# Routing logits on VectorE from replicated gate columns, k double-buffered, q and v single, and the last first-layer weights queued ahead of block 1

## What is computed

```python
# local attention: chunks of 32 queries, 16 keys to the left, 8 to the right, 8 memory keys
scores = scale * np.matmul(q_c, k_full.transpose(0, 1, 3, 2))
a = np.exp(scores - np.max(scores, axis=-1, keepdims=True))
a = a / (np.sum(a, axis=-1, keepdims=True) + 1e-09)
out[:, :, c_start:c_end] = np.matmul(a, v_full)
# dense feed-forward layer, 512 -> 2048 -> 512
h = x @ w_in
x = (h * (1.0 / (1.0 + np.exp(-h)))) @ w_out
# routed layer, 8 experts, one per token
logits = x @ w_gate + modality_bias[modality_id]
e_idx = np.argmax(logits, axis=1)
gate_w = softmax(logits)[e_idx]
out[mask] = gate_w * (np.maximum(x[mask] @ w1[e], 0.0) @ w2[e])
```

## Time and profile before

| | |
|---|---|
| median of 3 runs | 1012.25 us (1011.86 to 1015.44) |
| the profiled execution's own time | 1014.22 us |
| its span, first to last instruction | 1012.6 us |
| TensorE clock granted, mean share | 0.994 |
| TensorE, VectorE, ScalarE, GpSimd busy | 96%, 31%, 35%, 30% |

### The profile page before, as it was taken

How to read it: one execution, slowest core, us unless ns; L and a number is a source line. 1 busy time by engine, 2 the same in 40 slices (tenths; PEclk the granted TensorE clock), 3 DMA queues, 4 the chain that set the end, 5 groups by cost and what they waited for, 6 DMA issues and landing times.

```text
span 1012.6 us, 18134 instructions
## 1 busy us (share of the span) xinstructions
PE 976.3 (96%) x6148; PEld 842.9 (83%) x6149; DVE 309.1 (31%) x749; ACT 354.6 (35%) x728; POOL 302.9 (30%) x318
## 2 busy tenths in 40 slices
PE   4799999999999999999999999999999999999997
PEld 3688889889888888988888898988788888888875
DVE  4422323232422332332422221347332422222221
ACT  5655343343343343333344322343322322222221
POOL 4677222322232322232232234241122222222222
PEclk9999999999999999999999999998999999999999
DMA  7831021212322141242121002232511111111111
GB/s 265 306 105 55 25 78 40 71 47 72 65 47 79 57 57 40 63 49 78 56 56 55 1 33 63 83 94 33 199 54 37 44 38 42 42 42 42 42 42 44
DMA packets 31257, 69.35 MB, mean 68 GB/s; under 512 B 5343, under 2 KB 9439, under 8 KB 31168
## 3 DMA queue, kind: packets, MB, share of 16 engines
q1 hardware_dynamic: 22064, 48.29, 17.0%
q0 software_dynamic: 5904, 13.57, 4.5%
q10 hardware_dynamic: 3200, 6.34, 2.0%
HBM read 55.43 MB, written 13.02 MB: 68 GB/s over the span
## 4 chain that ended last, share of the span: by engine, by line
PE 91%; DMA 3%; DVE 2%; issue 1%; ACT 1%; POOL 1%; ACTq 0%; SPq 0%; POOLq 0%; DVEq 0%
PE bank L1261 26%; PE bank L1247 25%; PE bank L1458 14%; PE bank L1327 13%; PE bank L1232 2%; PE bank L1208 2%; PE bank L1469 2%; DMA q_in<-q_t 2%; PE bank L1292 2%; PE bank L1218 1%; PE bank L1316 1%; PE bank L1275 1%; DMA token_lists<-token,slot 1%; DVE row_sum L888 0%; ACT q_bd L637 0%
## 5 line engine op out<-in xcount | busy, mean ns | idle before, releaser
L578 POOL TENSOR_TENSOR g_lo<-g_raw,g_hi 128x384 fp32r<-128x384 f32 x128 | 131.3, 1026 | 412.0 <-ACT g_hi L771 400.5
L734 ACT ACTIVATE sig<-bank 128x384 f32<-128x384 f32 x128 | 62.8, 491 | 352.2 <-PE bank L1247 352.1
L904 DVE SCALAR_TENSOR_TENSOR g_raw<-sig,bank 128x384 f32<-128x384 f32 x128 | 70.9, 554 | 368.8 <-ACT sig L734 359.0
L1247 PE MATMUL bank<-x_hi,w_hi 128*128 128x384 f32 x512 | 177.7, 347 | 0.0
L1247 PE MATMUL bank<-x_hi,w_lo 128*128 128x384 f32 x512 | 173.2, 338 | 0.0
L1247 PE MATMUL bank<-x_lo,w_hi 128*128 128x384 f32 x512 | 172.1, 336 | 1.1 <-issue 1.1
L1261 PE MATMUL bank<-w_hi,g_hi 128*128 128x512 f32 x384 | 157.0, 409 | 3.1 <-POOL g_lo L578 3.1
L1261 PE MATMUL bank<-w_hi,g_lo 128*128 128x512 f32 x384 | 151.3, 394 | 0.0
L1261 PE MATMUL bank<-w_lo,g_hi 128*128 128x512 f32 x384 | 151.0, 393 | 0.0
L1247 PEld LDWEIGHTS bank<-x_hi,w_hi 128*128 128x128 f32 x512 | 96.5, 189 | 5.2
L1247 PEld LDWEIGHTS bank<-x_lo,w_hi 128*128 128x128 f32 x512 | 96.6, 189 | 3.2
(11 more groups left out here) (165 smaller groups left out, 1253.3 us busy)
## 6 DMA issues: line engine op xcount, KB each, us to landing
k_in<-k_ctx SPq DMA_DIRECT2D x32, 384.0 KB, 4.2
v_in<-v_ctx SPq DMA_DIRECT2D x32, 384.0 KB, 3.2
w_raw<-w SPq DMA_DIRECT2D x8, 1024.0 KB, 5.7
token_rows<-y_sb ACTq DMA_DIRECT2D x8, 774.0 KB, 3.9
q_in<-q_t SPq DMA_DIRECT2D x32, 192.0 KB, 3.1
w_raw<-w_in SPq DMA_DIRECT2D x4, 1024.0 KB, 6.9
w_raw<-w_out SPq DMA_DIRECT2D x4, 1024.0 KB, 8.6
list_id<-token_lists POOLq DMA_DIRECT2D x28, 0.5 KB, 2.3
```

The lines of the kernel that those rows point to most:

```text
L578: eng.tensor_tensor(g_lo[:, f % 2, :], g_raw[:, f % 2, :], g_hi[:, f % 2, :].bitcast(F32), ALU.subtract).then_inc(g_split, 1)
L734: eng.activation(sig[:, f % 2, :], h_bank[f % 2][:, 0:BLOCK], ACT.Tanh, scale=0.5)\
L904: eng.scalar_tensor_tensor(out=g, in0=s, scalar=1.0, in1=h_bank[f % 2][:, 0:BLOCK], op0=ALU.add, op1=ALU.mult).then_inc(g_done, 1)
L1247: mm = eng.matmul(h_bank[f % 2][:, 0:BLOCK], a, b, start=(k == 0 and n == 0), stop=(k == KC - 1 and n == 2))
```

## The change

- The routing logits of blocks 0 to 6 are computed by VectorE: `score(it, n)` multiplies a tile of y with one gate column that is replicated over all partitions (`wg_rows`, 128 x 8 x 512) and sums over the 512 elements, in one instruction and an accumulator read. There are 24 of them (3 tiles, 8 experts) in each of `it` = 2 to 8, three in each slot 3 to 10, each waiting for the one before, and they stand ahead of `silu` of their slot. `transpose_y`, `move_yt` and `logits` remain for the last block alone.
- `x_raw` is gone. `rest_of_x` moves from GpSimd to VectorE, which reads `o_bank` itself, behind `silu` of slots 3, 6, 9, 12; `values` waits for it (`x_split`) instead of for `x_hi_done`.
- `sig` is gone: tanh is written into `g_raw`, so it waits for the `g_lo` of two slots before (`g_split`) where `silu` did.
- q and v have one buffer (in block 0 parts of `wg_rows` serve as the second), k keeps two. Loads go in the order k, q of the next pair, then v of this one (`load_ahead`).
- Weight chunks 4 to 7 are queued ahead of the waiting loads of block 1, and behind those comes the load of `wg_rows`, 16 KB into each of 128 partitions (2 MB written).
- Some small tiles move to other memory, so `move_pt(0)` waits for `zero_stored` and `move_y` of `it` = 2 for `lists_cleared`.

The core of the diff:

```diff
-        q_in = early("q_in", [P, 2, BLOCK])
+        q_in = early("q_in", [P, BLOCK])
         k_in = early("k_in", [P, 2, CHUNKS * KEYS])
-        v_in = early("v_in", [P, 2, CHUNKS * HEAD_DIM])
+        v_in = early("v_in", [P, CHUNKS * HEAD_DIM])
+        wg_rows = early("wg_rows", [P, EXPERTS, D])
...
+        def pairs_before(blk, p):
...
+            return blk * PAIRS + p - (1 if blk * PAIRS + p <= PAIRS else 0)
...
             def load_q(blk, p):
-                need(eng, q_ready, 2 * (blk * PAIRS + p) - 2)
+                need(eng, q_ready, pairs_before(blk, p) * 2)
...
             def load_v(blk, p):
-                need(eng, pv_done, blk * PAIRS + p - 1)
+                need(eng, pv_done, pairs_before(blk, p))
...
-            load_v(1, 0)
-            load_pairs((1, 1),)
             for c in range(PAIRS, 2 * CHUNKS_W):
                 load_first(c)
+            load_ahead(1, 0)
+            eng.wait_ge(pv_done, PAIRS)
+            eng.dma_start(wg_rows[:, :, :], w_gate_t.partition_broadcast(P)).then_inc(rows_known, 16)
...
                 eng.wait_ge(pv_done, u + 1)
-                need(eng, x_split, u)
-                eng.activation(x_raw[:, :], o_bank[:, 0:BLOCK], ACT.Copy)
                 need(eng, l1_done, (it - 1) * FC)
                 eng.activation(x_hi[:, par, p, :], o_bank[:, 0:BLOCK], ACT.Copy).then_inc(x_hi_done, 1)
...
                         eng.wait_ge(l1_done, i + 1)
-                        need(eng, g_done, i - 1)
...
-                        eng.activation(sig[:, f % 2, :], h_bank[f % 2][:, 0:BLOCK], ACT.Tanh, scale=0.5)\
+                        need(eng, g_split, i - 1)
+                        eng.activation(g_raw[:, f % 2, :], h_bank[f % 2][:, 0:BLOCK], ACT.Tanh, scale=0.5)\
...
+            def rest_of_x(it, p, par):
+
+                eng.wait_ge(x_hi_done, it * PAIRS + p + 1)
+                eng.tensor_tensor(x_lo[:, par, p, :], o_bank[:, 0:BLOCK], x_hi[:, par, p, :].bitcast(F32), ALU.subtract)\
+                   .then_inc(x_split, 1)
...
+            def score(it, n):
+
+                t, e = divmod(n, EXPERTS)
+                if e == 0:
+                    eng.wait_ge(y_moved, (it - 2) * TT + (t + 1))
...
+                ins = eng.tensor_tensor_reduce(products[:, :], y_sb[:, t, 0:D], wg_rows[:, e, :], 1.0, 0.0, ALU.mult, ALU.add,
+                                               scored[:, t, e:e + 1])
+                ins.then_inc(score_step, 1)
...
+                    if route and ffn and 3 <= f < 3 + EXPERTS:
+                        for n in range((f - 3) * TT, (f - 2) * TT):
+                            score(it, n)
                     if route and f == 11:
                         route_choice(it)
...
                     if ffn:
                         silu(i, f)
+                    if attn and 1 <= p <= PAIRS and third == 0:
+                        rest_of_x(it, p - 1, par)
...
-                need(eng, x_hi_done, u)
+                need(eng, x_split, u)
...
-                    for t in tiles_at(it, f, 5) if route else ():
+                    for t in last_tiles(it, f, 5):
                         logits(it, t)
...
-                    for t in tiles_at(it, f, 3) if route else ():
+                    for t in last_tiles(it, f, 3):
                         transpose_y(it, t)
```

More of the change, by code:

```diff
@@ L247, in steps, with last_tiles @@
             step(BLOCKS + 1, 1, False, False, True, False)
[L249 to L253, removed]
+        def last_tiles(it, f, at):
+            return range(TT) if isinstance(it, int) and it == BLOCKS + 1 and f == at else ()
         def yt_bank(it, t):
-            return (pt_bank, *h_bank)[t] if isinstance(it, int) and it == BLOCKS + 1 else pt_bank
+            return (pt_bank, *h_bank)[t]
         def first_pieces(f):
@@ L274, in prob_of, with q_of, v_of @@
         def prob_of(it, p):
-            return y_t[:, 0, 0:TT, :].rearrange("p k s -> p (k s)") if doubled(it, p) else prob[:, :]
+            return wg_rows[:, 1, 0:BLOCK] if doubled(it, p) else prob[:, :]
+        def q_of(it, p):
+            return wg_rows[:, 0, 0:BLOCK] if doubled(it, p) else q_in[:, :]
+        def v_of(it, p):
+            return wg_rows[:, 2:4, :].rearrange("p e n -> p (e n)")[:, 0:CHUNKS * HEAD_DIM] if doubled(it, p) else v_in[:, :]
+        def pairs_before(blk, p):
+            if not isinstance(blk, int):
+                return blk * PAIRS + p
+            return blk * PAIRS + p - (1 if blk * PAIRS + p <= PAIRS else 0)
         def piece(to, i):
@@ L385, in _, with load_ahead @@
             load_first(3)
[L387 to L391, removed]
+            def load_ahead(blk, p):
+                if p < PAIRS - 1:
+                    load_k(blk, p + 1)
+                    load_q(blk, p + 1)
+                else:
+                    load_k(blk + 1, 0)
+                    load_q(blk + 1, 0)
+                load_v(blk, p)
             eng.dma_start(ids_sb[:, :, :], ids).then_inc(consts_loaded, 16)
@@ L470, in _ @@
             eng.memset(y_sb[:, :, D + 1:ROW], 0.0).then_inc(consts_made, 1)
-            eng.memset(zero_row, 0.0).then_inc(pool_step, 1)
             eng.iota(pad_ids, pattern=[[0, LIST // P]], base=PAD_TOKEN, channel_multiplier=0).then_inc(pool_step, 1)
-            eng.wait_ge(pool_step, 6)
+            eng.wait_ge(pool_step, 5)
             eng.dma_start(rows[TOKENS:TOKENS + 1, :], zero_row).then_inc(zero_stored, 16)
             eng.dma_start(lists.rearrange("(p n) a -> p (n a)", p=P), pad_ids).then_inc(lists_cleared, 16)
[L479 to L484, removed]
             def list_tokens(it, t):
@@ L748, in step @@
                             move_y(it, t)
-                    for t in tiles_at(it, f, 4) if route else ():
+                    for t in last_tiles(it, f, 4):
                         move_yt(it, t)
```

112 lines of the change are left out of this document (58 added, 54 removed).

## The result

The changed kernel takes 1002.3 us (median of 4 runs, 998.56 to 1004.66) against 1012.06 us (4 runs of the kernel before beside it, 1011.67 to 1015.44): the ratio is 0.9897, 95% interval 0.9867 to 0.9927. It is 1.0% faster, where 2.6% was forecast, and the time lies outside the range of 982.5 to 995. The profiled execution took 1000.61 us.

A forecast was written before the change was run, and what follows sets the result against it. TensorE, busy 976.3 of 1012.6 us, was taken as the bound. Terms -26.0 - 1.0 + 0.4 + 0.3 = -26.3 us against the median 1012.25 gave 986 us, 2.6% faster, range 982.5 to 995.

The forecast's parts named there:

- The transposes and logits taken off TensorE: On TensorE, slots 9 to 11: 1.24 us a tile removed for 21 tiles, 26.0 us gained (25 to 27.5).
- A score's price: On VectorE: 0.69 us plus 0.04 for the accumulator read, 0.73 us a score, bounded by 0.69 and 1.26.
- The rival with a second pass over the elements: VectorE becomes the bound: a score takes 1.26 us, so about 1033 us, slower than before; chance 0.08.
- VectorE's room, and the port: Three slots need 14.65 of 15.0 us on VectorE, including port contention with GpSimd, so VectorE just keeps pace.
- 2 us of locks: On VectorE, per three slots: scores and GpSimd's `g_lo` hold each other up at the shared port, counted as 2 us.
- the late q of (1, 2): At 56.23 us TensorE waits 1.02 us behind this late load; issuing the weights earlier removes it, -1.0 us.
- 0.3 us more: TensorE's waits for `g_lo`: margin 1.45 us against one lock of 0.7, priced at 0.3 us for the whole run.
- The 5 us that `silu` may be late: On VectorE: `silu` of slot f is wanted by `g_hi` at the end of slot f + 1, some 5 us later.
- the forecast's own formula: VectorE's need in three slots: 4.23 + 0.55 + 1.3 + 2 us plus the scores' price, against 15.0 us.
- The weights ahead: Loads at the start: -1.0 us for q of (1, 2), +0.4 (0 to 1.5) for q of (1, 1).
- a long wait for q, k or v at 40 to 50 us: Sign in the profile that would make the prediction wrong, at the loads of the start; no size given.
- the 0.05 that it shares with the ports: Rival that the gain is given back: stalls of 20 us or more from ports and late loads, 1007 to 1017; chance 0.05.

The follow-up runs named there:

- four scores: The changed kernel with four scores a slot instead of three, every third score computed twice: 997.83 us, ratio 0.9881 to the kernel before.
- Six scores: The changed kernel with six scores in every scoring slot instead of three, each computed twice: 1062.3 us, ratio 1.0528 to the kernel before.
- the version without both losses: The changed kernel with block 1's loads between the weight chunks and 16 empty instructions heading VectorE's program: 981.44 us, ratio 0.9726 to the kernel before.

## Why the prediction was wrong

**The transposes and logits taken off TensorE: right.** 26.0 us were summed. The slots 9 to 11 fell by 1.25 us, and the stretch between the marks by 27.93 us; 1.57 us of that are two waits at the turn of the loop (up to 354 and 357 us), which are under 0.45 us afterwards. These the sum didn't have, so that the middle came out over the 26.0 is in part luck.

**A score's price: right at the median.** 690 ns were forecast:

```profile
L925 DVE CUSTOM_DVE_ANT_0 products<-y_sb,wg_rows x168: 677/692/1528, 131.2 to 626.3; 128x512 f32<-128x512 f32 x168
...
L587 POOL TENSOR_TENSOR g_lo<-g_raw,g_hi x128: 987/1012/1512, 49.3 to 654.2; 128x384 fp32r<-128x384 f32 x128
```

The rival with a second pass over the elements falls: 512 elements cost 692 ns, about as much as the plain subtraction of the earlier trace rows (686). The Trainium skill's rule beside it (Vector Engine (DVE) Microarchitecture Reference, Points that are easy to get wrong) names the scalar-tensor-tensor form with two sources in SBUF that aren't bf16, at half rate. The score, a custom instruction in the trace with two such sources, doesn't show it.

**VectorE's room, and the port: right, with room to spare.** The forecast had 14.65 of 15.0 us: 11.35 us of work, 1.3 us behind `x_hi`, 2 us of locks. One stretch with nine scores, from one softmax to the next (with GpSimd's `g_lo` at its start):

```profile
362.08 0.56 DVE L882 TENSOR_REDUCE row_max<-bank 128x6 f32<-128x384 f32 x1
...
362.89 1.02 POOL L587 TENSOR_TENSOR g_lo<-g_raw,g_hi 128x384 fp32r<-128x384 f32 x1 [2.09 <-ACT g_hi L779]
363.15 1.31 DVE L925 CUSTOM_DVE_ANT_0 products<-y_sb,wg_rows 128x512 f32<-128x512 f32 x1
364.50 0.69 DVE L925 CUSTOM_DVE_ANT_0 products<-y_sb,wg_rows 128x512 f32<-128x512 f32 x1
365.23 0.69 DVE L925 CUSTOM_DVE_ANT_0 products<-y_sb,wg_rows 128x512 f32<-128x512 f32 x1
...
367.84 0.56 DVE L906 TENSOR_TENSOR x_lo<-bank,x_hi 128x384 fp32r<-128x384 f32 x1 [1.33 <-ACT x_hi L674]
...
362.08:377.06 14.98, 14.98 (x116) 13.12 (x115) 12.58 (x29) 5.62 (x13) 3.04 (x3) 1.00 0.28 67
```

12.58 us busy, locks included, and 1.33 us behind `x_hi`: 13.9 us, with 1.2 us of locks (12.58 - 11.35) where I took 2. The three scores show the lock: the first takes 1.31 us while `g_lo` runs (362.89 to 363.91), the next two 0.69. 37 of the 168 took over 0.8 us. TensorE waits for `g_lo` twice, 2.2 us in all, and for no score. Of the 3.1 us in the earlier trace rows, 1.02 are the late q of (1, 2), which the sum has as a term of its own; the other 2.1 became 2.2, where the sum had 0.3 us more. The 5 us that `silu` may be late were on the safe side. By the forecast's own formula, four scores need 4.23 + 0.55 + 1.3 + 2 + 12 x 0.73 = 16.8 of 15.0 us, over eight slots 4.9 us late, just inside the 5, and they cost nothing. Six scores need 21.2, 16.5 us late, which leaves 11.5 us of wait a step; 6.0 us of wait were measured, and 9.1 us of time (64 / 7). So the formula asks too much of VectorE, in the locks (1.2 us for 2) or in the lateness that is free; which of the two the runs don't tell. VectorE's busy time came to 471.6 us against the 450 forecast: the locks count as busy, and the mean score takes 849 ns.

**The weights ahead: the step that failed first.** The forecast had -1.0 for q of (1, 2), which went, and +0.4 (0 to 1.5) for q of (1, 1). It reasoned that q of (1, 1) "lands about when ScalarE wants it", from a rate of 4 MB in 12.25 us, as if the four chunks were all that is ahead of it. The trace of before had what that leaves out:

```profile
26.00:30.00 4.00, 1.75 (x25) 1.36 (x24) 2.59 (x5) 3.40 (x7) 1.72 (x3) 1.00 1.04 398
...
34.00:38.00 4.00, 3.59 (x51) 3.48 (x52) 1.18 (x3) 2.22 (x5) 0.00 (x0) 1.00 0.14 55
...
41.08 1.06 ACT L637 ACTIVATE q_bd<-q_in 64x384 f32<-64x384 f32 x2
```

ScalarE wants q of (1, 1) by 41.08. Before, chunks 4 to 7 are issued from 37.65 us on, when the DMA engines have run nearly empty (share 0.14), and the q behind them lands 14.75 us after the first of them. The change issues them from 25.32 on, 2.1 us behind chunks 2 and 3 (issued at 22.71 and 23.19), when the engines are full (1.04 even before the change). q lands at 46.15, 20.8 us after chunk 4. The 6.1 us more are what 2 MB take at the forecast's own rate (an estimate: 12.25 / 4 x 2), and chunks 2 and 3 are 2 MB. The wait can also be added up against its successor's in the earlier trace rows: q of (1, 1) is issued at 34.94 instead of 40.15, 5.2 us earlier, and lands 11.21 instead of 12.25 us later, but it is wanted at 46.17 - 5.83 = 40.34 instead of 50.9, 10.6 us earlier. So 1.50 - 5.2 - 1.04 + 10.6 = 5.9 us of wait, and 5.83 were measured. q was held up in being issued too: four of the issues ahead of it take 1.7 to 2.7 us each, where the chunks' issues took 0.4 to 0.5 before. And this wait carries the half clock with it: slots 0 and 1 of step 1 take 12.01 + 5.65 us instead of 5.94 + 4.60, 7.1 us more. Slots 2 and 3 take 10.35 instead of 11.62 us, where the wait of 1.0 us went, and slot 0 starts 0.4 us earlier: 7.1 - 1.3 - 0.4 is the +5.4 of the table. The text did name "a long wait for q, k or v at 40 to 50 us" as what would make it wrong, but gave it no price, and no chance beyond the 0.05 that it shares with the ports. No rival covers a time between 998 and 1007 us, where the result lies.

**The end: a term that was missing.** Nothing in the sum stood for VectorE's jumps behind the last product, and the change doesn't touch that code. It moved it: VectorE's program grew from 1882 to 2122 instructions. That cost 9.9 us, of which 16 empty instructions bring back 9.2 (15.36 - 6.12).

**What is left.** The sum was -26.3 us, and the version without both losses measures -28.3 us. The forecast failed on the two things beside the compute, not on what the change is about. What exactly decides whether a jump is long stays open. The place modulo 128 agrees with all fourteen kernels, but only five values of it were seen, four of the kernels ran once each, and it was read off the tail alone.

## What to carry to other kernels

When a bulk load is moved ahead of small ones, write down for the first small load behind it when it will be issued, what is still on its way then, when it lands and when it is wanted; put the small ones between the pieces of the bulk. A wait that leaves TensorE idle for some 5 us can also buy a stretch at half clock: here 5.8 us of wait cost 7.1. Before comparing two versions at the level of a per cent, look at what each engine does after its last instruction of work: a tail of skipped code moved the time by 1% here for a change of the code ahead of it, and a few empty instructions tell whether it does.

## What the runs showed of the hardware that was not expected

- The same jump of VectorE costs 0.2 to 0.3 us or 2.3 to 3.4 us (2.0 to 4.2 in the tails of all runs), by where the code stands. The packets of one instruction queue (q14) rise with the long ones (8 against 3 over the tail) and are 8 KB each (0.53 MB in 65 packets over the changed kernel). The Trainium skill has the mechanism (Runtime: NRT & Kernel Launch, Instruction fetch mechanics): an engine holds two pages of its code, and a taken branch to a target outside them waits for a fetch. The trace agrees, with a packet 0.5 to 0.6 us into each long jump of the two listings. It states pages of 16 KiB, which is 256 instructions. The packets of q14 are half of that (those of a second instruction queue, q8, have the 16 KiB), and the tail was short again 128 instructions on.
- An accumulating product of two fp32 tiles in SBUF takes 692 ns for 512 elements, no more than a subtraction of that size, and the read of its accumulator 81 ns, hidden all but 0.04 us.
- TensorE stood idle for 5.8 us from 41.5, and its granted clock was 0.50 (1.2 GHz) from 44.2 to 51.0, so it had fallen before the work came; in the kernel with six scores waits of 0.8 to 1.8 us were followed by half clock as well, for 3.4 us in each of six steps.
